# Splitting a step's weight set after its third chunk, moving token numbers, one high part and the loading of the out weights

## The chip, the core and the metric

The kernel runs on one core of a Trainium2 chip. A core has TensorE for matmuls, ScalarE, VectorE and GpSimd for element-wise work, and SyncE, which here only issues DMAs. The engines run their own instruction streams and wait for each other through semaphores. The metric is the device time of one execution in microseconds; lower is better.

## What is computed

Attention with exponential features, then a mixture of experts with one expert per token, then a gated feed-forward network (FFN). The reference, shortened:

```python
def phi(x):
    proj = np.einsum('bhsd,df->bhsf', x, w_phi)
    proj = proj - np.max(np.abs(proj), axis=-1, keepdims=True)
    return np.concatenate([np.exp(proj), np.exp(-proj)], axis=-1)
kv = np.einsum('bhsf,bhsd->bhfd', phi(k), v)
num = np.einsum('bhsf,bhfd->bhsd', phi(q), kv)     # divided by the same with v = 1
...
h = np.maximum(x[mask] @ w1[e], 0.0)               # per expert e: 512 -> 1024
out[mask] = gate_w[mask, None] * eom[mask, e, None] * (h @ w2[e])
...
xn = x / np.sqrt(np.mean(x * x, axis=-1, keepdims=True) + 1e-06) * rms_g
g = xn @ w_gate                                    # 512 -> 1536
return (g * (1.0 / (1.0 + np.exp(-g))) * (xn @ w_val)) @ w_out
```

4 batches of 576 positions give 2304 tokens of width 512; there are 8 experts. All data is float32.

## The kernel before

Each float32 operand of a large product is split into a high part (a float32r copy) and a low part (what is left), and a product is three matmuls: high by high, high by low, low by high. High parts are made by ScalarE, low parts by VectorE.

**Attention** takes the first 205 us, batch by batch. Tokens are scattered by expert into rows in DRAM (`xs_dram`, with the token's number in an extra column). The change does not touch this part.

**Experts' steps.** A step is one group of 288 tokens of one expert; with these inputs there are eight, numbered 0 to 7. Step 0 begins already while attention ends (the "early" step). In a step, TensorE makes eight chunks of hidden rows (`hidden`, 12 matmuls each) and adds each to the outputs (`outputs`, 12 matmuls each) two places later: h0 h1 h2 o0 h3 o1 h4 o2 and so on. Chunk m needs the low part of chunk m - 2, as does the output that follows it; a relu (ScalarE, L1376, into hmH) and its low part (VectorE, L1796, into hmL) are made per chunk. Behind chunk 4 TensorE multiplies the summed squares of the previous step by ones (`sum_squares`, L1149, named SS below), for the FFN's normalisation. These squares are GpSimd's (L782, L785, L788), which does in each step, in this order: three weight sums (L824, L828, L832), the squares, and the gating of the next group's rows (L775). VectorE then makes the mean (L1803), ScalarE the root (L1389), VectorE the inverse (L1808) and the normalised rows (L1817, `x2g`), which SyncE stores to `xn_dram`.

Beside this, each step of 1 to 7 prepares one set of the FFN's up weights (`t_raw`): SyncE loads it (L585, 512 KB), GpSimd forms sums in place, ScalarE makes the high part of the whole set (`weights_high`, L1399) and VectorE the low part (`weights_low`, L1929), and SyncE stores it to `t_dram` and loads the next. Steps 1 and 2 are each the first of an expert whose successor's weights have to be split as well: eight pieces, high by ScalarE (L1292), low by VectorE (L1736), two after chunk 1, two after chunk 2, one after chunk 4, two after chunk 5 and one at the end. GpSimd starts the loads of these weights (`w1raw`, `w2raw`, 2 MB each) once the pieces read from the buffer are done.

**FFN up.** Rows are taken in three groups of 768 tokens (`xst`, two halves of 384). For each block of weights (a visit) and group there is a unit, 36 in all: seven products of six matmuls (L1220 to L1222), whose weight and row operands include sums and differences of blocks (`s_sum`), so that seven products do the work of eight. Row operands are `sH` (ScalarE, L1488) and `sL` (VectorE, L1989). A unit's sums are copied by ScalarE (L1500, L1506, L1512), combined by VectorE (L1995, L2001 and L2009, `val`), pass a sigmoid (L1494) and two products (L2015, L2017) and are stored to `h_dram` (L634). The sigmoid of unit u waits for the store of unit u - 2, whose buffer it takes. Weights for visits 0 to 5 and 12 to 14 are read from `t_dram`, those of 6 to 11 are made on the spot.

**FFN out.** 18 tiles of 128 tokens, each 36 matmuls (L1271 to L1273) with the out weights `woH`, `woL`, split from `wo_st` during the last units by tables that name unit and place (A, B or C in a unit). Results are scattered to `out_dram` by token number (`ids_dram`, later `idI`).

**Order.** No scheduler decides it: each engine's stream is written out by hand, and the tables `OUT_HIGH_AT`, `OUT_LOW_AT`, `TILE0_HIGH_AT` and `TILE0_LOW_AT` hold places of the splits at the end. SyncE issues DMAs in program order and waits in that order. `rows_out(n)` stores a step's normalised rows and copies 288 token numbers of four bytes each from `xs_dram` to `ids_dram`.

Of the kernel before, what the change touches and what calls it, by code (L numbers as in the profile page):

```python
# [71 lines left out]
OUT_HIGH_AT = {(31, "C"): (0,), (32, "A"): (1, 2, 3), (33, "A"): (4, 5, 6), (34, "A"): (7, 8, 9), (35, "A"): (10, 11)}  # L72
OUT_LOW_AT = {(32, "A"): (0,), (32, "B"): (1, 2), (33, "A"): (3,), (33, "B"): (4, 5), (34, "A"): (6,), (34, "B"): (7, 8),
              (35, "A"): (9,), (35, "B"): (10, 11)}
TILE0_HIGH_AT = {(34, "C"): 0, (35, "C"): 1}
TILE0_LOW_AT = {(35, "A"): 0, (35, "C"): 1}
# [23 lines left out]
def build_program(nc, q, k, v, w_phi, wg, wog, w1, w2, ffn_up, ffn_out, rms_g, out):  # L100
# [9 lines left out]
    with ctx:  # L110
# [101 lines left out]
        wo_st = piece(0, 8)("wo_st", [P, NF, DM])  # L212
# [4 lines left out]
        hT_put = [placer(at_raw, 12288), piece(0, 4)]  # L217
# [5 lines left out]
        def sb(name, shape, dt=F32):  # L223
# [83 lines left out]
            "FFN rows loaded (one per group), their sums, operands split": "x_in0 x_in1 x_in2 s_add s_add1 s_hi s_lo",  # L307
# [6 lines left out]
            "FFN out weights loaded (in thirds), split": "wo_in0 wo_in1 wo_in2 wo_hi wo_lo",  # L314
# [163 lines left out]
        def _(e):  # L478
# [75 lines left out]

            e.wait_ge(s["tab_set"], 2)
# [12 lines left out]
            def rows_out(n):  # L568

                col, row = column_of(n), row_of(n)  # L570
                e.wait_ge(s["dve_xn"], n + 2)
                settle(e, "carry_sp")
                e.dma_start(xn_dram[:, :, bass.ds(col, G)], x2g[:, :, :]).then_inc(s["xst"], 16)
# [6 lines left out]
            def step_weights_in(n):  # L580

                nth = slice(n, n + 1) if isinstance(n, int) else bass.ds(step_number(n), 1)
                e.wait_ge(s["e_st"], n * 16 + 16)
                settle(e, "carry_sp")
                e.dma_start(t_raw[2][:, 0:4, :, :].rearrange("p o c n -> p (o c n)"),  # L585
                            ffn_up[nth].rearrange("a p n -> (a p) n")).then_inc(s["e_in"], 16)
# [10 lines left out]
            e.sem_inc(s["e_st"], 16)  # L597
            with e.If(early < 1):
                rows_in(row_of(0))
                step_weights_in(0)  # L600
                rows_next(1)
                weights_out(0)
            with e.If(early > 0):
                e.sem_inc(s["e_in"], 16)
                e.sem_inc(s["e_st"], 16)
            step_weights_in(1)
# [47 lines left out]
            rows_out(prior)  # L654
# [9 lines left out]
            for u in range(NU):  # L664
                hidden_out(u)
                if u == ROOT_AT + 1:
                    e.wait_ge(s["dve_xn"], total + 1)
                    settle(e, "carry_sp")
                    e.dma_start(xn_dram[:, :, bass.ds(last_col, G)], x2g[:, :, :]).then_inc(s["xst"], 16)
                if u == ROOT_AT + 2:  # L670
# [7 lines left out]
                if u == 8:  # L678
                    e.wait_ge(s["idst"], last * 16 + 16)
                    settle(e, "carry_sp")  # L680
                    with nc.allow_non_contiguous_dma(reason="token numbers"):
                        e.dma_start(ids_dram[bass.ds(last_col, G), :], xs_dram[bass.ds(last_row, G), DM:DM + 1])\
                            .then_inc(s["idst"], 16)
# [1450 lines left out]
```

## Time and profile before

| | us |
|---|---|
| median of 3 runs | 886.7 |
| lowest, highest | 885.47, 888.86 |
| the profiled execution | 884.25 |
| its span, first to last instruction | 882.5 |
| TensorE busy in it (the page's busy row) | 845.0 (96% of the span) |
| attention (to about) | 205 |
| experts' steps | 205 to 450 |
| FFN up | 451 to 732 |
| FFN out | 732 to 871 |

The stages are read from the timeline: the plain steps repeat every 27.2 us, a unit takes about 7.3 us and a tile 7.7 us. In the rows below, the bracket at the end of a timeline row is the time that the engine sat idle before that work and the event that ended the idleness. Times are from the start of the span.

### The profile page before, as it was taken

The page shows a single profiled execution, that of the slowest core. Times are in us where ns is not written, and L with a number is a line of the kernel's source. Part 1 is how long each engine was busy: PE and PEld are TensorE (multiplying, and loading weights), DVE is VectorE, ACT ScalarE, POOL GpSimd, SP SyncE. Part 2 cuts the span into 40 slices and gives each one's busy share as a digit, 9 for nine tenths or more (in the row PEclk, how much of TensorE's full clock was granted, in tenths as well). Part 3 has the DMA queues.
Part 4 walks back from the last instruction along what each step waited for, and adds up shares of the span by engine and source line. Part 5 has one row for each costly group of instructions (what it writes and reads, how often), then busy time and mean ns, then how long its engine had stood idle before and what let it go on. Part 6 is the DMA issues. An engine that isn't in the chain of part 4 may idle for free.

```text
span 882.5 us, 16593 instructions
## 1 busy us (share of the span) xinstructions
PE 845.0 (96%) x6216; PEld 764.6 (87%) x6217; DVE 527.9 (60%) x912; ACT 347.9 (39%) x548; POOL 186.9 (21%) x190
## 2 busy tenths in 40 slices
PE   8999999999979899999989999999999989999997
PEld 6686858678978899999978989999999988888886
DVE  5688888997555743445478777666765665122220
ACT  4555445662246333332254443333433433222211
POOL 1010303023263443424530031111110000111101
PEclk9999999999999899999999999999999999999999
DMA  8613714021647346554673852232222944343330
GB/s 284 205 55 151 257 53 161 2 77 35 261 166 221 136 132 144 103 126 138 179 175 126 275 182 78 78 79 78 78 78 58 390 161 167 131 143 112 128 107 36
DMA packets 65370, 122.41 MB, mean 139 GB/s; under 512 B 9216, under 2 KB 43136, under 8 KB 62496
## 3 DMA queue, kind: packets, MB, share of 16 engines
q1 hardware_dynamic: 57744, 91.98, 34.3%
q0 software_dynamic: 3488, 17.85, 5.3%
q10 hardware_dynamic: 4080, 11.80, 3.8%
q8 instruction: 37, 0.61, 0.3%
q14 instruction: 21, 0.17, 0.1%
HBM read 77.54 MB, written 44.09 MB: 138 GB/s over the span
## 4 chain that ended last, share of the span: by engine, by line
PE 78%; DVE 10%; DMA 5%; issue 5%; ACT 1%; POOL 0%; DVEq 0%; SPq 0%; POOLq 0%; ACTq 0%
PE ps L1220 9%; PE ps L1222 8%; PE ps L1221 8%; PE ps L1273 5%; PE ps L1271 5%; PE ps L1272 5%; PE ps L1128 3%; PE ps L1141 3%; PE ps L1129 3%; PE ps L1130 3%; PE ps L1142 3%; PE ps L1143 3%; PE ps L969 3%; PE ps L1024 3%; PE ps L929 2%
## 5 line engine op out<-in xcount | busy, mean ns | idle before, releaser
L1220 PE MATMUL ps<-sH,tb 128*128 128x384 f32 x504 | 171.8, 341 | 9.4 <-DVE val L2009 4.9
L1222 PE MATMUL ps<-sH,tb 128*128 128x384 f32 x504 | 170.6, 338 | 0.0
L1221 PE MATMUL ps<-sL,tb 128*128 128x384 f32 x504 | 170.6, 338 | 0.0
L1220 PEld LDWEIGHTS ps<-sH,tb 128*128 128x128 f32 x504 | 95.5, 190 | 12.4 <-DVE val L2009 6.6
L1221 PEld LDWEIGHTS ps<-sL,tb 128*128 128x128 f32 x504 | 95.7, 190 | 0.1
L1222 PEld LDWEIGHTS ps<-sH,tb 128*128 128x128 f32 x504 | 95.6, 190 | 0.0
L2027 DVE TENSOR_TENSOR hTL<-h_st,hTH 128x768 fp32r<-128x768 f32 x36 | 32.9, 954 | 97.4 <-ACT hTH L1528 97.4
L1128 PE MATMUL ps<-xmH,w1H 128*128 128x288 f32 x256 | 78.3, 306 | 13.2 <-DVE hmL L1796 9.3
L1796 DVE SCALAR_TENSOR_TENSOR hmL<-ps,hmH 128x288 fp32r<-128x288 f32 x64 | 29.1, 454 | 94.2 <-ACT hmH L1376 93.7
L1273 PE MATMUL ps<-woH,hTL 128*128 128x512 f32 x216 | 84.1, 389 | 0.0
L1272 PE MATMUL ps<-woL,hTH 128*128 128x512 f32 x216 | 84.1, 389 | 0.0
L1271 PE MATMUL ps<-woH,hTH 128*128 128x512 f32 x216 | 84.0, 389 | 0.0
L1141 PE MATMUL ps<-hmH,w2H 128*128 128x288 f32 x256 | 80.2, 313 | 0.0
L1129 PE MATMUL ps<-xmL,w1H 128*128 128x288 f32 x256 | 77.8, 304 | 0.0
L1130 PE MATMUL ps<-xmH,w1L 128*128 128x288 f32 x256 | 77.6, 303 | 0.0
L1142 PE MATMUL ps<-hmL,w2H 128*128 128x288 f32 x256 | 77.1, 301 | 0.0
L1143 PE MATMUL ps<-hmH,w2L 128*128 128x288 f32 x256 | 76.9, 300 | 0.0
L1376 ACT ACTIVATE hmH<-ps 128x288 fp32r<-128x288 f32 x64 | 26.3, 410 | 107.7 <-PE ps L1143 86.4
L899 POOL DMA_INDIRECT out_dram<-ysb,idI x18 | 17.5, 970 | 213.9 <-ACT ysb L1534 213.9
L1128 PEld LDWEIGHTS ps<-xmH,w1H 128*128 128x128 f32 x256 | 49.6, 194 | 15.0 <-DVE hmL L1796 10.2
L2015 DVE TENSOR_TENSOR hid<-hid,gate 128x768 f32<-128x768 f32 x36 | 35.8, 995 | 42.8 <-ACT hid L1494 42.7
L1594 DVE TENSOR_REDUCE mx<-ps 128x4 f32<-128x512 f32 x72 | 49.3, 685 | 17.8 <-PE ps L931 17.7
(245 smaller groups left out, 1772.4 us busy)
## 6 DMA issues: line engine op xcount, KB each, us to landing
h_dram<-hid SPq DMA_DIRECT2D x36, 384.0 KB, 2.7
h_st<-h_dram SPq DMA_DIRECT2D x18, 768.0 KB, 4.2
t_dram<-tb SPq DMA_DIRECT2D x6, 1792.0 KB, 5.7
t_raw<-in_ffn_up SPq DMA_DIRECT2D x13, 512.0 KB, 3.3
tb<-t_dram ACTq DMA_DIRECT2D x6, 1024.0 KB, 7.9
xin<-xs_dram SPq DMA_DIRECT2D x9, 578.2 KB, 9.0
xs_dram<-zrow SPq DMA_DIRECT2D x8, 578.2 KB, 7.9
qT<-in_q SPq DMA_DIRECT2D x4, 1152.0 KB, 5.7
```

The costliest lines, as they stand in the source:

```text
L1128: e.matmul(o, w1H[par][:, c, cols], xmH[:, c, :], start=(c == 0), stop=False)
L1129: e.matmul(o, w1H[par][:, c, cols], xmL[:, c, :], start=False, stop=False)
L1130: last = e.matmul(o, w1L[par][:, c, cols], xmH[:, c, :], start=False, stop=(c == KC - 1))
L1141: e.matmul(o, w2H[par][:, m, cols], hmH[:, m % 2, :], start=(m == 0), stop=False)
L1142: e.matmul(o, w2H[par][:, m, cols], hmL[:, m % 2, :], start=False, stop=False)
L1143: last = e.matmul(o, w2L[par][:, m, cols], hmH[:, m % 2, :], start=False, stop=(m == FC - 1))
L1220: e.matmul(to, wh, xh, start=(fresh and c == 0), stop=False, skip_group_check=True)
L1221: e.matmul(to, wh, xl, start=False, stop=False, skip_group_check=True)
L1222: done = e.matmul(to, wl, xh, start=False, stop=(c == 1), skip_group_check=True)
L1271: e.matmul(to, hi, woH[:, i, :], start=(i == 0), stop=False, skip_group_check=True)
L1272: e.matmul(to, hi, woL[:, i, :], start=False, stop=False, skip_group_check=True)
L1273: done = e.matmul(to, lo, woH[:, i, :], start=False, stop=(i == NF - 1), skip_group_check=True)
```

## The change

Six edits.

1. In a step, `weights_high` moves from behind relu 0 to behind relu 2 and its splits, `weights_low` from behind the low part of chunk 1 to behind that of chunk 3.
2. With an early step 0, SyncE issues the weight load of step 1 before it waits for the scatter and reads the table's other values.
3. `rows_out` is divided. The token numbers of the last step but one go out at unit 9 (after unit 8's store), those of the last at unit 11; the rows themselves go as before. The load of the third group's rows moves ahead of unit 5's store.
4. GpSimd's squares of the last step wait for the seventh low part of the first group's rows.
5. The first high part (`sH[0][0]`) is made by VectorE instead of ScalarE.
6. The out weights are staged in two halves in separate places, loaded at units 20 and 28; their splits and those of tile 0 have new places, and tile 0 and 1 change places in memory.

The diff, cut:

```diff
-OUT_HIGH_AT = {(31, "C"): (0,), (32, "A"): (1, 2, 3), (33, "A"): (4, 5, 6), (34, "A"): (7, 8, 9), (35, "A"): (10, 11)}
...
+OUT_HIGH_AT = {(30, "C"): (0, 1), (31, "A"): (2, 3), (31, "C"): (4,), (32, "A"): (5, 6), (33, "A"): (7, 8),
+               (34, "A"): (9, 10), (34, "C"): (11,)}
...
-        wo_st = piece(0, 8)("wo_st", [P, NF, DM])
+        wo_st = [placer(at_raw, 12288)("wo_st0", [P, NF // 2, DM]), piece(0, 4)("wo_st1", [P, NF // 2, DM])]
...
-        hT_put = [placer(at_raw, 12288), piece(0, 4)]
+        hT_put = [piece(4, 4), placer(at_raw, 12288)]
...
             e.wait_ge(s["c_pad"], 16 * E)
+            with e.If(early > 0):
+                e.sem_inc(s["e_in"], 16)
+                e.sem_inc(s["e_st"], 32)
+                step_weights_in(1)
             e.wait_ge(s["scat"], 16 * B * NJ)
             total = total_steps(e)
...
                 step_weights_in(n + 2)
-                rows_out(n)
+                col, row = column_of(n), row_of(n)
+                rows_out(n, col)
+                numbers_out(n, col, row)
...
-            rows_out(prior)
+            prior_col, prior_row = column_of(prior), row_of(prior)
+            rows_out(prior, prior_col)
...
                 if u == ROOT_AT + 1:
...
-                if u == ROOT_AT + 2:
+                    rows_out(last, last_col)
                     e.wait_ge(s["s_lo"], 7)
                     e.wait_ge(s["xst"], total * 16 + 32)
                     settle(e, "carry_sp")
...
                 if u == 8:
...
+                    numbers_out(prior, prior_col, prior_row)
+                if u == 10:
+                    numbers_out(last, last_col, last_row)
...
+                if u == 20:
+                    e.wait_ge(s["s_lo"], 7 * NSG)
+                    e.wait_ge(s["s_add"], 8)
+                    e.dma_start(wo_st[0][:, :, :], ffn_out[:, 0:NF // 2, :]).then_inc(s["wo_in0"], 16)
                 if u == last_of_group(0):
                     e.wait_ge(s["pe_D"], u + 1)
-                    for third in range(3):
-                        e.dma_start(wo_st[:, third * 4:third * 4 + 4, :], ffn_out[:, third * 4:third * 4 + 4, :])\
-                            .then_inc(s[f"wo_in{third}"], 16)
+                    e.dma_start(wo_st[1][:, :, :], ffn_out[:, NF // 2:NF, :]).then_inc(s["wo_in1"], 16)
...
             row_sums(0, 1)
+            e.wait_ge(s["s_lo"], 7)
             add_squares(total - 1)
...
                     if m == 0:
                         copy_out(g - 1)
-                        weights_high(g)
                     if split is not None:
                         for n in PIECES_AT.get(m, ()):
                             split(n)
+                    if m == 2:
+                        weights_high(g)
...
-                    if m == 1:
+                    if m == 3:
                         weights_low(g)
...
+            e.wait_ge(s["x_in0"], 16)
+            e.wait_ge(s["pe_s1"], total * FC)
+            settle(e, "carry_dve")
+            e.tensor_copy(sH[0][0][:, :, :], xst[0][:, 0:2, 0:GN]).then_inc(s["s_hi0"], 1)
             for o in range(4):
                 row_low(0, o)
```

ScalarE's stream at the start of a step with splits (steps 1 and 2); hmH is a relu, x2g the outputs copied, tb_95 the high part of the weight set, w1H_79 the splits. Before:

```order
L1376 ACTIVATE hmH<-ps 128x288
L1380 ISA
L1382 ISA
L1384 ACTIVATE x2g<-ps 128x1152
L1397 ISA
L1399 ACTIVATE tb_95<-t_raw_98 128x1792
L1374 REGISTER_ALU
L1376 ACTIVATE hmH<-ps 128x288
L1425 ISA
L1292 ACTIVATE w1H_79<-w1raw 128x1024 x2
```

and after:

```order
L1389 ACTIVATE x2g<-ps 128x1152
L1379 REGISTER_ALU
L1381 ACTIVATE hmH<-ps 128x288
L1431 ISA
L1297 ACTIVATE w1H_79<-w1raw 128x1024 x2
L1379 REGISTER_ALU
L1381 ACTIVATE hmH<-ps 128x288
L1297 ACTIVATE w1H_79<-w1raw 128x1024 x2
L1402 ISA
L1404 ACTIVATE tb_95<-t_raw_98 128x1792
L1379 REGISTER_ALU
L1381 ACTIVATE hmH<-ps 128x288
```

The set's high part now stands behind three relus and four splits, ahead of relu 3.

VectorE's stream from the low part of chunk 1 in the same step; hmL is a relu's low part, tb_95 the set's, w1L_80 the splits', and the row that writes rinv is the mean. Before:

```order
L1796 SCALAR_TENSOR_TENSOR hmL<-ps,hmH 128x288
L1927 REGISTER_ALU
L1929 TENSOR_TENSOR tb_95<-t_raw_98,tb_95 128x1792
L1935 ISA
L1935 COMPARE_AND_BRANCH
L1735 ISA
L1736 TENSOR_TENSOR w1L_80<-w1raw,w1H_79 128x1024
L1735 REGISTER_ALU
L1736 TENSOR_TENSOR w1L_80<-w1raw,w1H_79 128x1024
L1935 UNCONDITIONAL_BRANCH
L1795 REGISTER_ALU
L1796 SCALAR_TENSOR_TENSOR hmL<-ps,hmH 128x288
```

and after, from the splits of chunk 2:

```order
L1742 TENSOR_TENSOR w1L_80<-w1raw,w1H_79 128x1024
L1741 REGISTER_ALU
L1742 TENSOR_TENSOR w1L_80<-w1raw,w1H_79 128x1024
L1941 UNCONDITIONAL_BRANCH
L1801 REGISTER_ALU
L1802 SCALAR_TENSOR_TENSOR hmL<-ps,hmH 128x288
L1933 REGISTER_ALU
L1935 TENSOR_TENSOR tb_95<-t_raw_98,tb_95 128x1792
L1808 REGISTER_ALU
L1809 TENSOR_SCALAR rinv<-ps 128x288
```

The set's low part moved behind all four early splits and stands directly ahead of the mean.

SyncE's stream where the last step ends and the FFN begins; tb_94 are operands of visit 1, xst_100 the second group's rows. Before:

```order
L573 DMA xn_dram<-x2g 512x1x288
L574 ISA
L577 ISA
L577 DMA ids_dram<-xs_dram 288x1
L655 REGISTER_ALU
L618 DMA tb_94<-t_dram 128x2x1024
L618 DMA tb_94<-t_dram 128x2x768
L658 REGISTER_ALU
L629 DMA xst_100<-xn_dram 128x4x768
```

and after:

```order
L593 DMA xn_dram<-x2g 512x1x288
L662 REGISTER_ALU
L624 DMA tb_94<-t_dram 128x2x1024
L624 DMA tb_94<-t_dram 128x2x768
L665 REGISTER_ALU
L635 DMA xst_100<-xn_dram 128x4x768
```

The token numbers between the store of the rows and the operands are gone from here.

## Rows read from the trace of the kernel before

**Rows 1.** TensorE's waits: line, waited for, us in total, times, longest.
```profile
PE ps L1128 <- DVE hmL L1796: 9.3, 4, 3.4
PE ps L1220 <- DVE val L2009: 4.9, 4, 2.5
...
PE ps L1220 <- DVE sL L1989: 2.7, 3, 0.9
...
PE ps L1220 <- ACT part L1506: 1.8, 1, 1.8
```

**Rows 2.** Windows of 2 us: length, TensorE busy (instructions), clock, DMA share, GB/s.
```profile
252.00:254.00 2.00, 2.00 (x10) 0.50 0.01 4
...
450.00:452.00 2.00, 1.08 (x8) 1.00 0.97 47
...
706.00:708.00 2.00, 2.00 (x14) 1.00 1.02 400
...
718.00:720.00 2.00, 2.00 (x10) 0.71 0.00 0
```

**Rows 3.** Timeline of ScalarE: start, us, line, operation, idle before and its end.
```profile
248.47 1.70 ACT L1399 ACTIVATE tb<-t_raw 128x1792 fp32r<-128x1792 f32 x1 [4.14 <-POOL t_raw L832]
...
316.99 0.41 ACT L1376 ACTIVATE hmH<-ps 128x288 fp32r<-128x288 f32 x1 [1.54 <-PE ps L1143]
320.19 0.41 ACT L1376 ACTIVATE hmH<-ps 128x288 fp32r<-128x288 f32 x1 [2.79 <-PE ps L1143]
...
711.17 0.84 ACT L1494 ACTIVATE hid<-gate 128x768 f32<-128x768 f32 x1 [3.23 <-DMA h_dram<-hid]
```

**Rows 4.** Timeline of TensorE, step 1, the chunk behind the first hole.
```profile
251.01 0.40 PE L1128 MATMUL ps<-xmH,w1H 128*128 128x288 f32 x1 [3.40 <-DVE hmL L1796]
```

**Rows 5.** Timeline of VectorE, step 1 and the last step.
```profile
250.87 3.02 DVE L1929 TENSOR_TENSOR tb<-t_raw,tb 128x1792 fp32r<-128x1792 f32 x1
...
256.70 0.45 DVE L1796 SCALAR_TENSOR_TENSOR hmL<-ps,hmH 128x288 fp32r<-128x288 f32 x1
...
437.45 6.73 DVE L1817 SCALAR_TENSOR_TENSOR x2g<-x2g,gcol,rinv 128x288 f32<-128x288 f32 x4
```

**Rows 6.** Squares, splits and weight set by line: ns min/median/max, first and last start.
```profile
L782 POOL TENSOR_TENSOR sq<-x2g x8: 2107/2110/2171, 248.3 to 453.9; 128x1152 f32<-128x1152 f32 x8
...
L785 POOL TENSOR_TENSOR sq<-sq x8: 1422/3124/3129, 250.6 to 456.2; 128x576 f32<-128x576 f32 x8
...
L788 POOL TENSOR_TENSOR sq<-sq x8: 803/809/2370, 252.2 to 458.3; 128x288 f32<-128x288 f32 x8
...
L1736 DVE TENSOR_TENSOR w1L<-w1raw,w1H x12: 1211/1220/1822, 160.9 to 291.0; 128x1024 fp32r<-128x1024 f32 x12
...
L1929 DVE TENSOR_TENSOR tb<-t_raw,tb x7: 2012/2015/3024, 250.9 to 425.4; 128x1792 fp32r<-128x1792 f32 x7
```

**Rows 7.** The chain that ended last, in order of time: start, us, what.
```profile
232.14 0.27 SPq L429
...
233.79 11.28 DMA t_raw<-in_ffn_up
...
259.05 0.48 PE ps L1149 x2
...
293.17 0.96 PE ps L1149 x2
...
450.70 14.69 DMA xst<-xn_dram
...
696.27 14.82 DMA h_dram<-hid
```

**Rows 8.** Timeline of GpSimd, step 2, the first weight sum.
```profile
277.95 1.30 POOL L824 TENSOR_TENSOR t_raw<-t_raw 128x512 f32<-128x512 f32 x1 [1.51 <-issue]
```

**Rows 9.** Timeline of SyncE: DMAs issued (start, us of issuing, line).
```profile
445.49 0.62 SPq L577 DMA_DIRECT2D ids_dram<-xs_dram  x1
...
681.76 1.83 SPq L692 DMA_DIRECT2D wo_st<-in_ffn_out  x3
```

More of the change, by code:

```diff
@@ L306, in build_program @@
             "FFN up weights of a step: loaded, sums, operands split, stored": "e_in e_add e_hi e_lo e_st",
-            "FFN rows loaded (one per group), their sums, operands split": "x_in0 x_in1 x_in2 s_add s_add1 s_hi s_lo",
+            "FFN rows loaded (one per group), their sums, operands split": "x_in0 x_in1 x_in2 s_add s_add1 s_hi0 s_hi s_lo",
             "FFN up operands loaded (two parts per buffer)": "t_a0 t_a1 t_a2 t_b0 t_b1 t_b2",
@@ L313, in build_program @@
             "hidden rows stored (by group and buffer)": "h_o00 h_o01 h_o10 h_o11 h_o20 h_o21",
-            "FFN out weights loaded (in thirds), split": "wo_in0 wo_in1 wo_in2 wo_hi wo_lo",
+            "FFN out weights loaded (in halves), split": "wo_in0 wo_in1 wo_hi wo_lo",
             "a tile of hidden rows loaded (one per buffer), split in halves": "h_in0 h_in1 d_hi d_lo",
@@ L553, in _, with step_weights_in @@
                 rows_in(x0 * REGION + G)
+            def step_weights_in(n):
+                nth = slice(n, n + 1) if isinstance(n, int) else bass.ds(step_number(n), 1)
+                e.wait_ge(s["e_st"], n * 16 + 16)
+                settle(e, "carry_sp")
+                e.dma_start(t_raw[2][:, 0:4, :, :].rearrange("p o c n -> p (o c n)"),
+                            ffn_up[nth].rearrange("a p n -> (a p) n")).then_inc(s["e_in"], 16)
             e.wait_ge(s["tab_set"], 2)
@@ L566, in rows_next, with numbers_out @@
                 rows_in(row)
[L568 to L573, printed above, removed]
+            def numbers_out(n, col, row):
                 e.wait_ge(s["idst"], n * 16 + 16)
@@ L578, in rows_out @@
                         .then_inc(s["idst"], 16)
-            def step_weights_in(n):
-                nth = slice(n, n + 1) if isinstance(n, int) else bass.ds(step_number(n), 1)
-                e.wait_ge(s["e_st"], n * 16 + 16)
+            def rows_out(n, col):
+                e.wait_ge(s["dve_xn"], n + 2)
                 settle(e, "carry_sp")
-                e.dma_start(t_raw[2][:, 0:4, :, :].rearrange("p o c n -> p (o c n)"),
-                            ffn_up[nth].rearrange("a p n -> (a p) n")).then_inc(s["e_in"], 16)
+                e.dma_start(xn_dram[:, :, bass.ds(col, G)], x2g[:, :, :]).then_inc(s["xst"], 16)
             def weights_out(n):
@@ L602, in _ @@
                 weights_out(0)
[L603 to L606, printed above, removed]
+                step_weights_in(1)
             with e.Fori(0, total - 2) as n:
@@ L678, in _ @@
                 if u == 8:
[L679 to L683, printed above, removed]
+                    numbers_out(prior, prior_col, prior_row)
+                if u == 10:
+                    numbers_out(last, last_col, last_row)
                 if u == 15:
@@ L1550, in _ @@
             settle(e, "carry_act")
-            for o in range(4):
+            for o in range(1, 4):
                 row_high(0, o)
@@ L1985, in row_low @@
                        else x[:, 2:4, GN:2 * GN])
-                e.wait_ge(s["s_hi"], 7 * sg + o + 1)
+                if (sg, o) == (0, 0):
+                    e.wait_ge(s["s_hi0"], 1)
+                else:
+                    e.wait_ge(s["s_hi"], 7 * sg + o)
                 if o in (3, 5):
```

19 lines of the change are left out of this document (8 added, 11 removed).

## Prediction

> **What bounds the kernel.** I read the page's busy row first, then TensorE's waits, then the timeline around each wait, and last the clock in 2 us windows. TensorE is busy for 96% of the span (the table above), so only its holes and slow stretches can be won. Its waits name four families [rows 1]: the experts' steps (9.3 us in four waits for hmL), the start of the FFN (2.7 us in three waits for sL, 1.8 us for a sum on chip) and val (4.9 us in four waits). To each belongs a tail at the lower clock: of the 2 us windows from 230 to 880, twelve show a granted clock under 0.8; the first and the last of them are in [rows 2]. 0.50 is 1.2 GHz against the 2.4 GHz elsewhere, and every such stretch follows a hole of 1.6 to 3.4 us. Where matmuls run at half speed, half of that time is lost: about 1.7 us after the holes of step 1, 3.0 in step 2, 1.7 around 446 and 1.7 around 471, 1.8 at 716. Everything else runs without a hole, and the change does not touch its matmuls.
>
> **Weight sets in the steps.** Step 1 shows the hole: ScalarE starts the high part of the weight set at 248.47, after 4.14 us of idle time for GpSimd's sums, and only then does relu 1 [rows 3]; TensorE stands from 247.61 to 251.01 [rows 4]. Then VectorE does the set's low part in 3.02 us ahead of two splits, and the second hole comes before 256.70 [rows 5]. Step 2 repeats this. Together: 9.3 us of holes [rows 1] and 4.7 of clock, 14.0 us.
>
> After the change relu 1 and its low part are not held up, and these holes go. What is late next? TensorE reaches the matmul of the squares (L1149) behind chunk 4, and it needs GpSimd's three square instructions, which stand behind the three sums. In plain steps two chunks take 3.20 us (the distance of two relus, [rows 3]), so one takes 1.6, and with chunks 3, 1 and 4 following 247.61 without a hole TensorE asks at 252.4. When is GpSimd done? Its squares need 2.11, 1.42 and 0.81 us when nothing is beside them, but the last took up to 2.37, the second up to 3.13; VectorE's weight set took 2.01 or 3.02, its splits 1.22 or 1.82 [rows 6]. The pattern in both directions is that one finishes before the other starts: step 1's 3.02 us began at 250.87 [rows 5], in a square instruction.
>
> The Trainium skill, "SBUF — State Buffer", section "Who interferes with whom", says that a VectorE instruction with two SBUF inputs and a GpSimd instruction that reads SBUF exclude each other, the second to issue being blocked until the first ends. By that rule, the trace agrees (2.01 against 3.02, 0.81 against 2.37); with no exclusion at all the squares would end near 252 and the gain would be the first rival's.
>
> Before, VectorE was idle during the sums (ScalarE stood still), so they ran in 3.2 us. Now four splits of 1.22 fall among sums and squares. By hand, with the load landing at 243.8 (below): first sum to 245.2, second to 246.1; splits 0 and 1 to 248.5; third sum to 249.2; splits 2 and 3 to 251.5; first square to 253.6; weight set to 255.6; second square to 257.0; third to 257.9. The matmul of the squares runs at 258.0 instead of 259.05 [rows 7]: 1.05 us won, although the old holes are gone, because one hole of 5.6 us has taken their place. After it a slow stretch is due that the old kernel had ahead of that matmul: minus 1.7. Step 1 gives **-0.65 us**. ScalarE's high part (1.70 us, [rows 3]) now stands behind four splits and ahead of relu 3; it waits for nothing there but the third sum and hides in TensorE's new hole.
>
> Step 2 starts its sums at 277.95 [rows 8], held by GpSimd's weight load, which waits for the last split of step 1, so its phase stays. The same count gives: sums to 283.2, squares to 292.1. The matmul of the squares then comes at 292.2, not 293.17 [rows 7]: +1.0. Before, 2.9 us of slow clock lay behind it (1.45 lost); now a slow stretch of 1.7 does. Step 2: **+0.75**. In the five plain steps there are no splits. The low part (2.01) moves between relu 3's low part and the mean, delays the mean by about 1 us and relu 4 by 0.2, against about 2 us of slack in a 3.2 us period: nothing. Both unknown sizes stay open: with VectorE and GpSimd taking turns one by one the two steps gain up to 4, with slow stretches of 3.0 they lose 3.
>
> **Early load.** SyncE issued step 1's weights at 233.79, after reading table values from 232.14 on [rows 7]; the issue now stands ahead of those reads, so about 1.3 us earlier. The load needed 11.28 us beside two 2 MB loads of GpSimd; the bounds of what is won at its end are 0 and, if it gets ahead of the second one, some 5 us. I take the 1.3, since nothing overtakes in these rows: landing at 243.8.
>
> **Token numbers.** SyncE issues 288 four-byte pieces at 445.49 [rows 9], and behind them the operands and the rows xst1. The DMA engines are 0.97 busy at 47 GB/s then [rows 2], and the rows need 14.69 us from 450.70 [rows 7]. Without them some 0.6 MB of rows, 1.8 MB of operands and 1.5 MB of xst1 are in the queue, at the 400 GB/s of a full window [rows 2] about 9.5 us from 445, so xst1 lands near 456.5, before unit 1 asks at 459. The 1.8 us hole and its 1.7 us tail go. In units 9 and 11 the same pieces delay only stores that have a unit of slack (7.3 us against 8), and one such transfer is at that place already.
>
> **First high part, and squares after the seventh low part.** VectorE makes the first high part while ScalarE is still in its table load, at most 0.95 us as its low parts; the first of the three 0.9 us holes goes. With GpSimd's squares held back until the seventh low part, the other two go as well: 2.7 us. What is late next: the squares now run at 457.6 to 462.3 beside VectorE's row sums of unit 1, each waits for the other, and by the same count TensorE stands 1.15 us before product 5 of unit 1 and 0.85 before unit 1's last product. 2.7 + 1.8 + 1.7 - 2.0 = **+4.2**; bounds 2 (a slow stretch on top) and 6.2.
>
> **Out weights.** Three loads, 3 MB, went out at 681.76 [rows 9] in front of operand and hidden loads; the store of hidden rows at 696.27 landed after 14.82 us instead of 2.7 [rows 7], and ScalarE's sigmoids waited 3.23 us [rows 3]. TensorE stood 2.5 us [rows 1] and lost 1.8 at the lower clock [rows 2]. Half of the bytes, 1.57 MB, is now loaded in unit 20, when the DMA engines are mostly idle; at 400 GB/s the store lands 3.9 us earlier, 0.7 more than the wait. The splits are spread over more units, at no more than two a place, into engines with over 2 us free a unit. **+4.4**; bounds 0 and 4.4.
>
> **Sum.** -0.65 + 0.75 + 4.2 + 4.4 = 8.7 us. The profiled execution took 884.25 (span 882.5), so 875.55. The median of the runs, 886.7, stands 2.45 above it; against that scale 878.0 us.
>
> **Rivals.**
> (1) GpSimd's squares are ready in time: GpSimd gets ahead of the splits, or the early load overtakes GpSimd's second one. The holes before L1149 shrink to 1 or 2 us. For: the load is small. Against: the load of 11.28 us showed no overtaking. Then the steps give back 14.0 - 3.6 = 10.4 instead of 0.1: 867.7 us.
> (2) The store of hidden rows still lands after the sigmoids are due, since its margin is 0.7 us and operand loads of 1.8 MB are issued after it: the 4.4 stay. 882.4 us.
> (3) The slow stretches after the two long holes last as in step 2 before (3.0 rather than 1.7) and the start of the FFN gets one too: 878.0 + 2.6 + 1.7 = 882.3 us.
> (4) On the other side: in the plain steps the weight set now stands ahead of the mean, and ScalarE waits for the root behind it before relu 4. If it met GpSimd's gating as x2g's four products met GpSimd's row sums at 437 (6.73 us, [rows 5], for four instructions of the kind that takes 0.45 in hmL's row: 3.7 times), it would take 7.5 us and relu 4's low part would miss chunk 6 by 3.4 us. It decides against the kernel from about 4 us of low part upwards. With a slow stretch after each, five steps cost 5 x (3.4 + 1.7) = 25: 903 us. Against it: in plain steps the squares end before relu 3 and gating is 2.0 us of short instructions, of which at most one is in the way.
> (5) The changed order doesn't do what it says: the load lands at 245 all the same. Then step 1 is 1.2 us worse: 879.2, in the forecast's range.
>
> **How the numbers follow.** Forecast with (5) 0.57, (1) 0.15, (2) 0.12, (3) 0.12, (4) 0.04. A measurement here tells some 0.5% (4.4 us) from no change, that is below 882.3 or above 891.1. The forecast and (1) are faster, (2) and (3) lie on the border: faster 0.79, same 0.17, slower 0.04. The range takes in (1), (2) and (3): 867 to 883.
>
> **What would show it.** In the profile after: TensorE's longest wait in steps 1 and 2 is at L1149's line for GpSimd, 5 to 6 us each, and no longer for hmL; the rows' load lands within 7 us of its issue and no wait for part at the FFN's start; no wait of the sigmoids for the hidden store, no slow window at 716. Wrong would be: step 1 with a hole of 2 us or less (rival 1), a store of over 11 us (2), any hole in a plain step (4).

## The result and the profile after

| | before | after |
|---|---|---|
| median, us | 887.8 (4 runs, 885.5 to 890.0) | 877.2 (4 runs, 875.3 to 878.0) |
| ratio after to before | | 0.988 (95% interval 0.985 to 0.991) |
| profiled execution: span | 882.5 | 873.7 |
| step 1 begins (its relu 0) | 242.85 | 247.99 |
| steps 1 and 2 (relu 0 to relu 0) | 34.14 + 35.10 = 69.2 | 31.03 + 30.98 = 62.0 |
| start of step 3 to the end of the span | 570.4 | 563.7 |

The forecast of 878.0 us was met, but not by its own terms: the steps gave 7.2 us in these two executions where it had 0.1, the rest gave 6.7 where it had 8.6, and attention, whose code nobody touched, took 5.1 us back. Relu 0 of steps 1, 2 and 3 after, from which the stages are read:

```profile
247.99 0.41 ACT L1381 ACTIVATE hmH<-ps 128x288 fp32r<-128x288 f32 x1 [1.82 <-PE ps L1135]
...
279.02 0.41 ACT L1381 ACTIVATE hmH<-ps 128x288 fp32r<-128x288 f32 x1 [0.95 <-PE ps L1135]
...
310.00 0.41 ACT L1381 ACTIVATE hmH<-ps 128x288 fp32r<-128x288 f32 x1 [1.96 <-PE ps L1135]
```

TensorE's waits after, answering [rows 1] (line, waited for, us in total, times, longest); lines shifted with the edits, so that L1133 is the hidden product, L1225 a unit's product, L1154 the matmul of the squares, L1029 a part of attention:

```profile
PE ps L1029 <- issue: 4.0, 9, 0.8
...
PE ps L1225 <- DVE val L2018: 2.9, 5, 1.5
...
PE ps L1225 <- DVE sL L1998: 2.4, 1, 2.4
...
PE ps L1146 <- ACT x2g L1389: 1.4, 1, 1.4
PE ps L1133 <- DVE hmL L1802: 1.3, 2, 1.1
...
PE ps L1154 <- POOL sq L792: 0.8, 1, 0.8
```

The 9.3 us for hmL are 1.3, and no 5 to 6 us wait for the squares came in their place. One wait of 2.4 for sL stands where three of 0.9 stood (the same kernel before, profiled once more below, has one of 2.4 and two of 0.9). A wait for x2g is new.

GpSimd in step 1 after (start, us, line); its sums, squares and turns with VectorE:

```profile
248.49 1.30 POOL L828 TENSOR_TENSOR t_raw<-t_raw 128x512 f32<-128x512 f32 x1 [11.46 <-DMA t_raw<-in_ffn_up]
...
250.89 0.74 POOL L836 TENSOR_TENSOR t_raw<-t_raw 128x256 f32<-128x256 f32 x1 [0.18 <-POOL t_raw L832]
251.59 3.09 POOL L786 TENSOR_TENSOR sq<-x2g 128x1152 f32<-128x1152 f32 x1
...
257.22 1.55 POOL L792 TENSOR_TENSOR sq<-sq 128x288 f32<-128x288 f32 x1 [0.18 <-POOL sq L789]
```

and VectorE's four splits beside them:

```profile
250.99 4.77 DVE L1742 TENSOR_TENSOR w1L<-w1raw,w1H 128x1024 fp32r<-128x1024 f32 x2 [0.49 <-ACT w1H L1297]
...
256.05 3.81 DVE L1742 TENSOR_TENSOR w1L<-w1raw,w1H 128x1024 fp32r<-128x1024 f32 x2
```

The first sum starts 0.50 us after relu 0; before, the load landed at 245.07 ([rows 7]), 2.2 us after relu 0 at 242.85. All three sums run at their own length, the third beginning just ahead of the first split (250.89 and 250.99). Then squares and splits take turns one by one: two splits take 4.77 instead of 2.44. The squares end 10.8 us after relu 0; the forecast had 15.1.

The windows that answer to [rows 2] (2 us each: length, TensorE busy, weight loads, VectorE, ScalarE, GpSimd, clock, DMA share, GB/s):

```profile
256.00:258.00 2.00, 1.82 (x12) 1.64 (x12) 2.00 (x2) 1.04 (x2) 1.82 (x2) 1.00 0.00 0
258.00:260.00 2.00, 1.22 (x8) 1.07 (x8) 2.00 (x3) 0.00 (x0) 2.00 (x2) 1.00 0.00 0
...
450.00:452.00 2.00, 2.00 (x9) 2.00 (x8) 1.66 (x2) 2.00 (x4) 0.00 (x0) 0.55 1.03 415
452.00:454.00 2.00, 2.00 (x9) 2.00 (x8) 1.56 (x3) 0.47 (x1) 0.00 (x0) 0.59 0.98 388
...
712.00:714.00 2.00, 2.00 (x14) 2.00 (x12) 1.86 (x3) 1.69 (x4) 0.00 (x0) 1.00 0.00 0
...
716.00:718.00 2.00, 2.00 (x13) 2.00 (x12) 1.42 (x2) 0.46 (x2) 0.00 (x0) 1.00 0.00 0
```

Between 230 and 868 us only two windows show a clock under 0.8, against twelve before. That is one execution of each: in others there are four after (a_same) and seven before (b_same).

### The profile page after: what moved, and what is told of

The parts are those of the page before. It is cut to its first block, busy times and chain, and to the rows that moved or that the text cites. A ratio compares the mean times of both kernels' runs of the same rounds, so it can differ in the third digit from the quotient of the medians.

```text
span 873.7 us, 16594 instructions
## 1 busy us (share of the span) xinstructions
PE 840.9 (96%) x6216; PEld 758.6 (87%) x6217; DVE 526.3 (60%) x913; ACT 347.5 (40%) x547; POOL 177.9 (20%) x190
## 4 chain that ended last, share of the span: by engine, by line
PE 79%; DVE 10%; issue 6%; DMA 2%; ACT 1%; DVEq 0%; SPq 0%; POOLq 0%; POOL 0%; ACTq 0%
PE ps L1225 9%; PE ps L1227 9%; PE ps L1226 9%; PE ps L1276 5%; PE ps L1278 5%; PE ps L1277 5%; PE ps L1029 3%; PE ps L1133 3%; PE ps L974 3%; PE ps L1134 3%; PE ps L1135 3%; PE ps L1146 3%; PE ps L1148 3%; PE ps L1147 3%; PE ps L934 2%
## 5 line engine op out<-in xcount | busy, mean ns | idle before, releaser
L1225 PE MATMUL ps<-sH,tb 128*128 128x384 f32 x504 | 171.1, 340 | 6.1 <-DVE val L2018 2.9
L1225 PEld LDWEIGHTS ps<-sH,tb 128*128 128x128 f32 x504 | 95.0, 189 | 9.0 <-DVE val L2018 5.5
L1133 PE MATMUL ps<-xmH,w1H 128*128 128x288 f32 x256 | 76.3, 298 | 5.3 <-issue 3.1
L1512 ACT ACTIVATE part<-ps 128x384 f32<-128x384 f32 x36 | 17.7, 493 | 110.6 <-PE ps L1227 107.5
```

Of the source, the lines that this page charges most:

```text
L1133: e.matmul(o, w1H[par][:, c, cols], xmH[:, c, :], start=(c == 0), stop=False)
L1225: e.matmul(to, wh, xh, start=(fresh and c == 0), stop=False, skip_group_check=True)
```

## The measure: stages instead of whole times

The executions of one kernel differ by up to 10 us, so that most edits of 1 to 5 us don't show in a ratio. A profile says where a difference lies, so the experiments are read by stage. A label with a_ is the changed kernel with something taken back or added, b_ the kernel before, c_ a new version. Each stage below is read from one profiled execution. The medians of different rows don't compare directly, since the kernel before, timed beside them, had 887.8 us beside after, 890.4 beside a_wset, a_num, a_out and a_sqcast, 887.0 beside b_same, b_wset, a_early and c_rowsfirst, and 886.8 beside the others; the ratios do.

| kernel | median, us | ratio to before (95%) | relu 0 of step 1 | step 1 + step 2 | step 3 to end |
|---|---|---|---|---|---|
| before | 887.8 | | 242.85 | 34.1 + 35.1 | 570.4 |
| b_same | 885.7 (1 run) | | 248.18 | 34.4 + 33.1 | 568.3 |
| b_wset | 885.1 | 0.997 (0.994 to 1.000) | 246.67 | 35.8 + 31.3 | 567.2 |
| after | 877.2 | 0.988 (0.985 to 0.991) | 247.99 | 31.0 + 31.0 | 563.7 |
| a_same | 878.6 | 0.989 (0.985 to 0.993) | 250.51 | 31.0 + 31.6 | 563.8 |
| a_wset | 882.5 | 0.991 (0.987 to 0.994) | 251.75 | 33.6 + 33.9 | 562.5 |
| a_early | 878.9 | 0.990 (0.985 to 0.994) | 248.54 | 34.8 + 29.9 | 564.5 |
| a_num | 882.4 | 0.988 (0.984 to 0.993) | 251.89 | 30.9 + 32.2 | 566.2 |
| a_out | 881.4 | 0.989 (0.985 to 0.994) | 247.51 | 30.9 + 32.4 | 567.4 |
| a_sqcast | 877.1 | 0.986 (0.983 to 0.990) | 247.36 | 31.0 + 31.8 | 562.8 |
| a_twice | 882.6 (1 run) | | 250.27 | 33.5 + 32.6 | 564.5 |
| c_rowsfirst | 875.8 | 0.988 (0.983 to 0.992) | 248.36 | 30.1 + 30.2 | 562.4 |
| c_start | 874.6 | 0.987 (0.981 to 0.993) | 247.46 | 30.0 + 31.3 | 561.1 |
| c_squares_first | 874.9 | 0.984 (0.979 to 0.988) | 248.90 | 29.9 + 28.6 | 567.5 |

A stage repeats to about 0.6 us in after and a_same, to 2 us in before and b_same. A stretch of TensorE at the lower clock, which comes in one execution and not in another, makes 1.4 to 1.7 us in most cases (the lost time summed over windows of 2 us), so a difference below 2 us between two stages shows little by itself; where one is used below, the waits behind it are given too.

## Experiments

**The kernel before, once more (b_same).**

> The kernel before once more, unchanged, for one profile. In the profiled execution of before, step 1 begins (its relu 0) at 242.85 us; in those of the changed kernel and of four kernels made from it at 247.4 to 251.9, with waits for issue in attention's L1029 that before lacks, though attention's code is the same. Theory A: this differs from run to run: step 1 begins here at 246 or later. Theory B: the changed program does it: 243 again and no such waits.

Theory A. TensorE's waits in it:

```profile
PE ps L1128 <- DVE hmL L1796: 6.8, 3, 3.6
...
PE ps L1024 <- issue: 4.3, 8, 1.0
```

Step 1 begins at 248.18. The profiled execution of before was the exception among 14, the others lie between 246.7 and 251.9; so the 5 us are not the change's doing. That it adds one or two is not excluded: before, b_same and b_wset have 242.9, 248.2 and 246.7, the kernels made from the changed one 247.4 to 251.9. Why attention's length varies stays open.

The waits for sL in b_same are those of a kernel without edits 4 and 5 (it has 2.42, 0.92 and 0.86):

```profile
PE ps L1220 <- DVE sL L1989: 4.2, 3, 2.4
```

In before the first of them was only 0.92, and TensorE had run slowly just ahead of it; the same pair is in c_rowsfirst (0.91, behind windows at 0.72 and 0.50). The lower clock took 1.7 us there, and the wait was 1.5 shorter. The windows of before:

```profile
446.00:448.00 2.00, 2.00 (x11) 0.53 1.11 266
448.00:450.00 2.00, 2.00 (x12) 0.62 1.08 82
```

**The weight set's place: taken back (a_wset), alone (b_wset).** a_wset, and b_wset the same with the signs turned, in the kernel before:

```diff
                     if m == 0:
                         copy_out(g - 1)
+                        weights_high(g)
...
-                    if m == 2:
-                        weights_high(g)
...
-                    if m == 3:
+                    if m == 1:
                         weights_low(g)
```

> The changed kernel with edit 1 alone taken back (high part of the weight set behind relu 0, low part behind that of chunk 1). Theory A (the traces): the order of the weight set is what freed steps 1 and 2, by 3.1 and 4.1 us between two relus 0, so this kernel is about 7 us slower than the changed one (about 884), step 1 is 34 us long again with two holes of over 3 us before hmL, and GpSimd's squares are later beside a 3 us weight set. Theory B (the forecast): the order is worth 0.1 us, since one late square takes the place of the holes: 877 to 878. Theory C: the steps were freed by the earlier load of the weights, not by the order: under 2 us slower and step 1 still near 31 us.

> The kernel before with edit 1 alone (high part of the weight set behind relu 2, low part behind that of chunk 3). Theory A: taking it back cost 2.5 and 2.9 us of steps 1 and 2, so adding it gives the same: steps of 31.6 and 32.2 us instead of 34.1 and 35.1, the kernel 5.4 us faster than before. Theory B: edit 1 gives more only together with the early load, whose sums it needs: under 2 us.

Taken back, the waits for hmL return and the two steps take 67.4 us, 5.4 more than after and 4.8 more than a_same. That is theory A in kind, with less than its 7 us and with no hole over 2.7; B and C fell:

```profile
PE ps L1133 <- DVE hmL L1801: 8.7, 4, 2.7
```

Added alone, the same edit is worth little: 67.1 us against 69.2 and 67.5, ratio 0.997. The waits for hmL are gone, and the forecast's long waits for the squares are there. TensorE's waits and GpSimd's step 1 in b_wset:

```profile
PE ps L1149 <- POOL sq L788: 8.4, 2, 6.0
```

```profile
249.59 1.29 POOL L824 TENSOR_TENSOR t_raw<-t_raw 128x512 f32<-128x512 f32 x1 [13.87 <-DMA t_raw<-in_ffn_up]
251.05 1.50 POOL L828 TENSOR_TENSOR t_raw<-t_raw 128x256 f32<-128x256 f32 x1 [0.18 <-POOL t_raw L824]
252.73 1.50 POOL L832 TENSOR_TENSOR t_raw<-t_raw 128x256 f32<-128x256 f32 x1 [0.18 <-POOL t_raw L828]
254.20 3.09 POOL L782 TENSOR_TENSOR sq<-x2g 128x1152 f32<-128x1152 f32 x1
```

Two sums take 1.50 here instead of 0.74: the load came 2.9 us after relu 0, and they fell among the splits. Theory B holds for b_wset: the order needs the earlier load. The early load alone in the kernel before was not run; a_wset has it without the new order, and its two steps take 67.4 us, no better than b_wset.

**The early load (a_early).**

```diff
                 e.sem_inc(s["e_st"], 32)
-                step_weights_in(1)
             e.wait_ge(s["scat"], 16 * B * NJ)
...
                 weights_out(0)
-                step_weights_in(1)
+            step_weights_in(1)
```

> The changed kernel with edit 2 alone taken back: step 1's weight load is issued after the table's values. Theory A: sums and squares of step 1 are 1.3 us later; TensorE waited only 0.8 us for the squares, so step 1 grows by about 1.3 us to 32.3, all else alike: 1.3 us slower. Theory B: since the load still lands when GpSimd's two of 2 MB have gone, it lands at the same distance from relu 0 and nothing changes: under 0.5 us in step 1.

Both were too small: step 1 takes 34.8 us, 3.8 more, with the hole that the forecast had drawn:

```profile
PE ps L1153 <- POOL sq L791: 8.1, 2, 5.7
```

The issue of step 1's load in after and in a_early (relu 0 at 247.99 and 248.54):

```profile
237.60 0.36 SPq L561 DMA_DIRECT2D t_raw<-in_ffn_up  x1
...
239.51 0.36 SPq L561 DMA_DIRECT2D t_raw<-in_ffn_up  x1
```

Issued 9.0 us ahead of relu 0, the load lets GpSimd begin 2.6 after it; issued 10.4 ahead, 0.5 after it. So 1.35 us of earlier issue gave 2.1 of earlier landing, and the squares ended 4.4 us earlier. Step 2 gives 1.1 to 1.6 of it back: the store of the rows is issued 7.5 us ahead of the next relu 0 in after (271.55), 9.6 ahead in a_early (273.74), and only the first is waited for (below). Side by side, TensorE's wait for the squares against what GpSimd did:

| where | first sum, after relu 0 | squares end, after relu 0 | TensorE waits |
|---|---|---|---|
| after, step 1 | 0.5 | 10.8 | 0.8 |
| b_wset, step 2 | 1.0 | 12.0 | 2.4 |
| a_early, step 2 | 1.0 | 12.0 | 2.4 |
| c_rowsfirst, step 2 | 1.3 | 12.3 | 2.7 |
| a_early, step 1 | 2.6 | 15.2 | 5.7 |
| b_wset, step 1 | 2.9 | 15.5 | 6.0 |

Each GpSimd instruction that falls among the splits takes 0.7 to 1.0 us more than alone, less than the 1.22 of one split, and never the 2.44 of two. (The last square of b_wset's and a_early's step 1, 2.35 instead of 0.81, ran beside the low part of the weight set.)

**One square more (a_twice).**

```diff
                 settle(e, "carry_pool")
+                if twice:
+                    e.tensor_tensor(sq[:, :, :], x2g[:, :, :], x2g[:, :, :], ALU.mult).then_inc(s["pl_dup"], 1)
+                    e.wait_ge(s["pl_dup"], n + 2)
+                    settle(e, "carry_pool")
```

> The changed kernel with GpSimd forming the first squares of a step twice (one more instruction, 2.1 us alone, 3.1 beside splits). Theory A: the gain of steps 1 and 2 is the distance of GpSimd's last square from relu 0, and TensorE has less than 1 us of slack there: squares of step 1 end 13.5 to 14 us after relu 0 instead of 10.8, the hole ahead of the squares' matmul grows from 1 to about 4 us, step 1 takes 34 us and step 2 some 33.5; plain steps stay at 27.2. Theory B: GpSimd gets its turns faster when it has more to do, or another wait is the later one: steps grow by under 1 us.

Theory A. The squares of step 1 end 13.7 us after relu 0, and

```profile
PE ps L1159 <- POOL sq L796: 4.6, 2, 3.8
```

Plain steps stay at 27.2 us. In step 1 the squares end 2.9 us later, TensorE waits 3.0 more for them, and the step takes 2.5 more: GpSimd's last square sets the pace of step 1, nearly one for one. In plain steps 2 us more of GpSimd's work are free.

**The token numbers (a_num).**

```diff
             rows_out(prior, prior_col)
+            numbers_out(prior, prior_col, prior_row)
...
-                if u == 8:
-                    numbers_out(prior, prior_col, prior_row)
```

> The changed kernel with the token numbers of the last step but one copied again right behind its rows at the start of the FFN. Theory A: the second group's rows land after unit 1 asks for them, as before, with a wait of some 1.8 us and a low clock behind it: 3.5 us slower (about 880.7), load of the rows over 12 us. Theory B: in the changed kernel other waits at that place (sL, the row sums of VectorE) are the later ones, so the load may be late without cost: under 1 us slower.

Theory A. ScalarE waits for the second group's rows, issued at 451.89, and the clock drops behind the hole:

```profile
468.32 1.58 ACT L1493 ACTIVATE sH<-xst 128x768 fp32r<-128x768 f32 x2 [4.50 <-DMA xst<-xn_dram]
```

```profile
PE ps L1224 <- ACT part L1511: 2.9, 1, 2.9
```

```profile
472.44:474.44 2.00, 2.00 (x9) 2.00 (x8) 1.97 (x4) 0.49 (x1) 0.00 (x0) 0.54 0.04 8
```

From step 3 to the end it takes 2.5 us more than after and a_same, and has two slow stretches where each of them has one. In the 44 us around the FFN's start, summed over 2 us windows, TensorE loses 6.5 us in holes and 3.4 at the lower clock; after loses 4.8 and 1.7, a_same 4.5 and none.

**The out weights (a_out).**

```diff
-                if u == 20:
...
-                    e.dma_start(wo_st[0][:, :, :], ffn_out[:, 0:NF // 2, :]).then_inc(s["wo_in0"], 16)
...
-                    e.dma_start(wo_st[1][:, :, :], ffn_out[:, NF // 2:NF, :]).then_inc(s["wo_in1"], 16)
+                    for third in range(3):
+                        e.dma_start(wo_st[:, third * 4:third * 4 + 4, :], ffn_out[:, third * 4:third * 4 + 4, :])\
```

(with the four tables and both placements of before)

> The changed kernel with the out weights in one place again, loaded in three parts at unit 28, with the old tables and places of tiles 0 and 1. Theory A: a hidden store lands after some 15 us, the sigmoids wait over 3 us for it, a hole of 2.5 us and a low clock follow: 4.4 us slower (about 881.6). Theory B: the wait was a matter of the phase of the stores against the loads, and a kernel whose FFN begins some 8 us earlier but with the same units meets it in the same way only in part: under 2 us slower.

Theory A: 3.7 us more from step 3 to the end, the hole of 2.9 us back with a low clock. TensorE's wait, ScalarE's sigmoid, and the store in the chain:

```profile
PE ps L1222 <- DVE val L2015: 5.8, 5, 2.9
```

```profile
706.89 0.84 ACT L1497 ACTIVATE hid<-gate 128x768 f32<-128x768 f32 x1 [3.67 <-DMA h_dram<-hid]
```

```profile
691.55 15.26 DMA h_dram<-hid
```

In after the stores of that time took 4.3 to 9.6 us, and no sigmoid waited.

**First high part and held squares (a_sqcast).**

```diff
-            e.wait_ge(s["s_lo"], 7)
             add_squares(total - 1)
...
-            for o in range(1, 4):
+            for o in range(4):
                 row_high(0, o)
...
-            e.tensor_copy(sH[0][0][:, :, :], xst[0][:, 0:2, 0:GN]).then_inc(s["s_hi0"], 1)
```

> The changed kernel with edits 4 and 5 taken back: the first high part by ScalarE, the last squares not held back. Theory A (the forecast's terms): the two edits remove 2.7 us of waits for sL and add 2.0 in unit 1, so 0.7 us slower, with three waits of some 0.9 us for sL at the start of the FFN and squares ending before unit 1. Theory B (the trace after, where one wait of 2.4 us stands in place of three of 0.9): the two edits are worth nothing or cost up to 2 us, since the squares beside the row sums of unit 1 are gone from there: 875 to 877.

Not decided: the waits for sL are again those of b_same (2.5, 0.9 and 0.9, in all 4.3 us), the two holes in unit 1 (0.50 and 0.59 in after) are gone, and from step 3 to the end it takes 562.8 against 563.7 and 563.8. By the number that is theory B. But after and a_same each have a slow stretch of 1.7 us there and a_sqcast has none; TensorE's holes in the FFN's first 44 us are 5.8 against 4.8 and 4.5, which is nearer to the 0.7 of theory A. VectorE's two low parts with the squares beside them again (1.82 in after), and its first high part in after:

```profile
452.73 4.11 DVE L1994 TENSOR_TENSOR sL<-s_sum,sH 128x768 fp32r<-128x768 f32 x2
```

```profile
447.50 0.56 DVE L2073 CAST sH<-xst 128x768 fp32r<-128x768 f32 x1 [3.09 <-issue]
```

ScalarE made its own first high part at 447.25. VectorE stood 3.09 us on nothing that the profile shows, so handing it this one gained nothing: the first wait for sL is 2.4 in after and 2.5 here. The two edits were taken back only together.

**The rows' store ahead of the next load (c_rowsfirst).** The new wait, ScalarE's copy of the outputs in step 2 of after, and SyncE's order that made it:

```profile
282.43 1.13 ACT L1389 ACTIVATE x2g<-ps 128x1152 f32<-128x1152 f32 x1 [3.00 <-DMA xn_dram<-x2g]
```

```profile
262.53 0.39 SPq L600 DMA_DIRECT2D t_dram<-tb  x1
269.59 0.36 SPq L561 DMA_DIRECT2D t_raw<-in_ffn_up  x1
271.55 0.71 SPq L593 DMA_DIRECT2D xn_dram<-x2g  x1
```

The low part of the weight set comes later, and so does its store (14.5 us after relu 0, 262.53; before 11.3, 254.14). The next load waits for that store, and the rows, which were ready at 268.9, are issued behind the load. The edit:

```diff
                 weights_out(n + 1)
-                step_weights_in(n + 2)
                 col, row = column_of(n), row_of(n)
                 rows_out(n, col)
+                step_weights_in(n + 2)
```

> The changed kernel with SyncE storing the normalised rows ahead of the next weight load in the steps, instead of behind it. Theory A: in step 2 the outputs' copy waits 3.0 to 4.4 us for that store, which stands behind the weight store and the weight load; ahead of the load it goes 2 us or more earlier, the wait shrinks below 1 us and TensorE's 1.4 to 2.8 us for x2g go: step 2 at 29.5 instead of 31.0 to 32.4, 1.5 to 3 us faster. Theory B: the store is late because of what it shares the DMA engines with, not because of its place: no change, or step 3 loses by a later weight load what step 2 gains.

Theory A in its mechanism, with less gained: the wait for the store is gone, the steps take 60.3 instead of 62.0 and 62.6 (theory A had 29.5 for step 2, 30.2 came). But step 2's load now comes 1.3 us after relu 0 and TensorE waits there for the squares:

```profile
PE ps L1154 <- POOL sq L792: 3.5, 2, 2.7
```

**Two new versions (c_start, c_squares_first), beside the changed kernel once more (a_same).**

> The changed kernel once more, unchanged, as the measure for the two new versions beside it and for how much its stages differ from run to run. Both theories: steps 1 and 2 together 62 to 63.5 us, last relu 0 to the end 431 to 433, the ratio to before 0.987 to 0.990.

It came as expected: 62.6 us for the steps, ratio 0.989. The edit of c_start, on top of that of c_rowsfirst:

```diff
             row_sums(0, 0)
+            e.wait_ge(s["dve_xn"], total)
+            settle(e, "carry_pool")
             e.wait_ge(s["e_lo"], total)
...
-            e.wait_ge(s["s_lo"], 7)
+            e.wait_ge(s["s_lo"], 6)
             add_squares(total - 1)
```

> A new version: the changed kernel with the rows' store ahead of the next weight load in the steps (as tried), GpSimd's last two row sums of the first group waiting until VectorE has made the normalised rows of the last step but one, and the last squares held back until the sixth low part instead of the seventh. Theory A: VectorE's four products at the end of the last step, 6.4 us beside GpSimd's sums, shrink to under 4.5, the hole of 1.2 us there goes, and the squares end before the row sums of unit 1, whose hole of 0.5 us goes: 1.5 to 2 us faster than with the store's place alone, last relu 0 to the end near 430. Theory B: the row sums now end when sH needs them, and what is gained at the step's end is lost at the FFN's start: within 0.5 us.

Theory A, a little less: VectorE's four products at the end of the last step take 3.37 us, not 6.43, the holes of 1.3 us behind them and of 0.50 in unit 1 are gone, and from step 3 to the end the kernel has the shortest time of all, 561.1, 1.3 less than c_rowsfirst, at 61.3 us for the steps. By stages it is 3 to 4 us ahead of after; by whole times (874.6 against 878.6 beside it) the intervals overlap.

```profile
434.16 3.37 DVE L1825 SCALAR_TENSOR_TENSOR x2g<-x2g,gcol,rinv 128x288 f32<-128x288 f32 x4
```

c_squares_first is c_start with, in addition:

```diff
             def split_step(pair, par, g):
-                weight_sums(g)
                 add_squares(g - 1)
+                weight_sums(g)
...
-                    if m == 2:
+                    if m == (2 if split is None else 4):
                         weights_high(g)
```

(and the low part behind chunk 5 in steps with splits)

> A second version: as the first, and in steps with splits GpSimd makes the squares ahead of the weight sums, the weight set's high part is made behind relu 4 and its low part behind that of chunk 5. Theory A: squares no longer wait for the load of the weights, end some 7 us after relu 0, before TensorE asks at 9.8, and the holes ahead of the squares' matmul (1 to 2.7 us) go in both steps: steps 1 and 2 together 57 to 58 us instead of 60.3, 2 to 3 us faster than the first version. Theory B, the other side: the weight set now crowds VectorE behind chunk 5 or the next load comes too late for step 3, whose sums start late: the steps give back less than 1 us in all.

Both theories in part: steps 1 and 2 take 58.5 us and never wait for the squares, but from step 3 to the end it takes 6.4 us more than c_start. GpSimd's new order also runs in step 6 (the first of its expert, without splits), where ScalarE kept its place:

```profile
399.25 1.70 ACT L1406 ACTIVATE tb<-t_raw 128x1792 fp32r<-128x1792 f32 x1 [4.27 <-POOL t_raw L836]
```

From there the store (403.91), the next load (410.43) and the last step's sums (420.17) are late, and TensorE stands 2.0 us at the squares, with a low clock behind. A second low stretch at 522 adds to the 6.4; no row explains it. The median of 874.9 is no worse than c_start's. A version with the order kept apart for that step was not run.

## Why the prediction was right, and where not

**Weight sets: the total 0.1 was wrong, by 6 us.** Two sizes failed in the count of step 1: "first sum to 245.2, second to 246.1; splits 0 and 1 to 248.5", and the landing at 243.8 from which it starts. First, turns: for sums that start 1.0 us after relu 0 the count gave an end at 15.1; b_wset and a_early measured 12.0. It let VectorE do two splits for each GpSimd instruction; the rows show one. Second, the landing: 1.3 us of earlier issue were carried over as 1.3, and 2.1 came, which put all sums ahead of the splits: 12.0 became 10.8. The text had seen that both unknowns were open ("taking turns one by one the two steps gain up to 4"), and even that bound was too low. Rival 1 is what happened in step 1, by its own sign of a hole of 2 us or less; it over-priced the gain at 10.4 (6 measured), in part since step 2 got a new wait for the rows' store that no term had (c_rowsfirst, without it, takes 1.7 to 2.3 us less). Other short waits that before doesn't have are in the two steps of after: 1.0 for nothing that the profile shows, 0.8 and 0.5 for xmL. The count also had a low clock of 1.7 us behind the squares in each step; after has none in either step, a_same 1.5 in step 2. Of a step that was moved, the DMA behind it and what SyncE had queued behind that were not counted.

By the rule of the Trainium skill, "SBUF — State Buffer", section "Who interferes with whom", that a GpSimd instruction which reads SBUF and a VectorE instruction with two SBUF inputs contend, and that the order of issue decides which of them blocks, the traces agree: 0.74 against 1.50 for a sum among splits.

**Early load: priced at 1.3, worth 3.8 in step 1** (a_early), 2.1 to 2.7 with what step 2 gives back, and nearly all of it only with the weight set moved (a_wset, which has the load without the new order, takes 67.4 us for the steps, before and b_same 69.2 and 67.5). Rival 5 fell.

**FFN start: 4.2 forecast, about 2.7 measured** (holes and low clock in those 44 us: 9.5, 7.4 and 7.4 in before, b_same and b_wset, 6.5, 4.5, 6.2 and 4.6 in after, a_same, a_wset and a_early; a_out and a_twice, with the same code there, have 4.9 and 6.5). The token numbers are nearly all of it (2.5 in a_num, one slow stretch of 1.7 more included); the rows' load landed after 8.6 us, not within 7, in time all the same. The 2.7 for edits 4 and 5 was wrong: the first high part came no earlier, and the wait for it stayed at 2.4 as in b_same; only the two of 0.9 behind it went, as forecast. The holes in unit 1 came, at 0.5 and 0.6 instead of 1.15 and 0.85. And the 1.7 us of low clock around 446 in before, which the text had among the losses (in no term of its sum), were hardly lost, as far as four executions show: the wait behind it was shorter by 1.5.

**Out weights: 4.4 forecast, 3.7 measured** in a_out. The mechanism was as described; the low clock behind the hole, counted at 1.8 always, is there in some executions only. Rival 2 fell (stores up to 9.6 us).

**Slow stretches (rival 3).** Its two long holes didn't come. The stretch that it has for the FFN's start is there in after (450 to 454, 1.7 us) and not in a_same. **Plain steps (rival 4)** stayed at 27.2 us: the low part ran in 2.02 us.

**The sum.** Leaving attention out, the profiles of before and b_same take 639.7 and 635.8 us, of after and a_same 625.7 and 626.4: 11.7 us on average, not 8.7: 6.1 in the steps instead of 0.1, 5.6 behind them instead of 8.6. The median fell by 10.6. That the forecast met the time to 1 us is luck: the steps were 6.0 us too low, the rest 3.0 too high, and the median of before stood 1 us higher in the end than the one it was reckoned from. The terms behind the steps don't add up exactly either: 2.7 and 3.7 by their own measures are 6.4, not 5.6; the difference is within what a stage repeats to.

## What to carry to other kernels

When a step is moved past others, follow the chain of queues that its result starts (here store, load, the next store in the same queue) into the next period. Where two engines exclude each other, count one instruction of each in turn, and look at how many instructions fall before the other engine begins: sums that began 0.5 us earlier ended the squares 1.2 us earlier. Two edits may be worth about 1 us each alone (b_wset 67.1, a_wset 67.4 against 68.4 on average of before and b_same) and 6 together (62.3), so undo them one by one from the finished kernel as well as adding them one by one.

## What was not expected of the hardware

The clock after a hole is not a function of the hole. In b_wset TensorE stood for 2.7 us at the place of val and ran on at full clock; in before a hole of 2.5 us at the same place ([rows 1]) brought a clock of 0.50 to 0.71 ([rows 2] has its end). The first window behind it in before, then b_wset's wait and windows:

```profile
716.00:718.00 2.00, 2.00 (x8) 0.50 0.24 71
```

```profile
PE ps L1220 <- DVE val L2010: 5.4, 5, 2.7
```

```profile
712.00:714.00 2.00, 0.38 (x3) 0.06 (x1) 1.92 (x2) 2.00 (x5) 0.00 (x0) 1.00 0.62 187
714.00:716.00 2.00, 0.92 (x5) 0.92 (x6) 1.94 (x3) 0.28 (x1) 0.00 (x0) 1.00 1.03 353
716.00:718.00 2.00, 2.00 (x14) 2.00 (x13) 1.66 (x4) 0.53 (x2) 0.00 (x0) 1.00 0.18 53
```

So a profile's low-clock time is one draw. Behind a hole TensorE lost nothing (b_wset's 2.7), 1.4 us (a_early's 5.7) or 3.0 us (b_same's 3.6), summed over windows of 2 us: no run here shows what decides it. Attention's length, 242.9 in one execution and 246.7 to 251.9 in thirteen others of the same code there, is another draw: a span read from one execution carries several microseconds whose cause no run here shows.
